# Attention's cluster chain on DVE in three pieces, x rows turned a head later; an expert up projection with the weights stationary and 256 tokens moving

## The reference, cut to what matters

```python
# attention: batch 2, 8 heads, 768 positions, 64 dims, 16 clusters per head
q_assign = argmax(einsum(q_n, c_n)); k_assign = argmax(einsum(k_n, c_n))
mask = q_assign[:, :, :, None] == k_assign[:, :, None, :]
scores = where(mask, scale * q @ k.T, -1e9)
x = softmax(scores) @ v                      # rearranged to (1536, 512)
# dense block: d_model 512, d_ff 1024
h = x @ w_in
solu = h * softmax(h)
x = (layernorm(solu) * g_ln) @ w_out
# experts: 8 experts, w1 (512, 1024), w2 (1024, 512), top 1, capacity 384
expert_idx = argmax(x @ w_gate); gate_w = softmax(x @ w_gate)[expert_idx]
h = maximum(disp @ w1, 0)
y = h @ w2
out[i] = gate_w[i] * y[expert_idx[i], pos[i]]
```

## Time and profile before

| | |
|---|---|
| median of 3 runs | 747.68 us (745.71 to 748.03) |
| the profiled execution, its own time | 743.6 us |
| its span | 741.8 us |
| mean granted TensorE clock | 0.956 |
| PE, DVE, ACT, POOL busy, share of the span | 86%, 60%, 56%, 39% |
| bytes by DMA, mean rate | 86.08 MB, 116 GB/s |
| the costliest DVE groups | p_lo 192 of 547 ns, maximum 96 of 954 ns |

### The profile page before, as it was taken

One profiled execution on the slowest core, in us unless ns is written; L12 is line 12 of the kernel. 1 busy time (PEld: TensorE's weight loads), 2 busy tenths in 40 slices (PEclk: granted clock), 3 DMA queues, 4 the chain that ended last, 5 costly groups with the idle time before them and its releaser, 6 DMA issues. The chain is left out here.

```text
span 741.8 us, 12378 instructions
## 1 busy us (share of the span) xinstructions
PE 640.7 (86%) x4272; PEld 560.7 (76%) x4272; DVE 444.5 (60%) x773; ACT 418.6 (56%) x772; POOL 292.4 (39%) x277
## 2 busy tenths in 40 slices
PE   2888999999999899579999999734999999999983
PEld 2778888888888889468888888633777887877862
DVE  5688887888788788346656465351635616346430
ACT  3577877787778788435453545310645627446630
POOL 3457676667767656464332010003022312314211
PEclk9999999999999999789999999975999999999997
DMA  4745454545454530071120000007547535367200
GB/s 119 206 118 151 120 152 116 132 117 151 108 142 102 136 87 2 15 271 42 43 85 14 28 15 15 28 15 258 172 164 274 191 129 208 125 237 248 73 18 14
DMA packets 37378, 86.08 MB, mean 116 GB/s; under 512 B 6719, under 2 KB 8895, under 8 KB 37314
## 3 DMA queue, kind: packets, MB, share of 16 engines
q1 hardware_dynamic: 33474, 75.78, 34.4%
q0 software_dynamic: 3840, 9.45, 3.9%
HBM read 53.74 MB, written 12.58 MB: 89 GB/s over the span
## 5 line engine op out<-in xcount | busy, mean ns | idle before, releaser
L437 DVE TENSOR_TENSOR p_lo<-t_ps,p_hi 128x384 f16<-128x384 f32 x192 | 103.7, 547 | 17.4 <-ACT p_hi L328 15.5
L432 DVE TENSOR_REDUCE neg_max<-s_ps 128x1 f32<-128x768 f32 x96 | 91.6, 954 | 32.4 <-PE s_ps L531 31.9
L328 ACT ACTIVATE p_hi<-t_ps 128x384 f16<-128x384 f32 x192 | 89.9, 488 | 31.9 <-PE t_ps L542 29.3
L531 PE MATMUL s_ps<-KK,QQ 128*128 128x384 f32 x384 | 94.0, 368 | 0.0
L554 PE MATMUL pv_ps<-v_cut,p_hi 128*128 128x192 bf16 x576 | 91.5, 248 | 0.7 <-ACT pv_sb L328 0.5
L542 PE MATMUL t_ps<-consts,p_exp 128*128 128x128 f32 x576 | 90.8, 277 | 1.4 <-ACT p_exp L352 0.8
L1238 POOL DMA_INDIRECT out<-y,info x24 | 26.5, 1105 | 164.3 <-ACTq L1179 78.3
L555 PE MATMUL pv_ps<-v_cut,p_lo 128*128 128x128 bf16 x576 | 89.1, 221 | 0.0
L352 ACT ACTIVATE p_exp<-s_ps,neg_max 128x768 f32<-128x768 f32 x96 | 87.0, 906 | 1.7 <-DVE neg_max L432 1.7
L542 PEld LDWEIGHTS t_ps<-consts,p_exp 128*128 128x128 f32 x576 | 71.7, 146 | 7.9 <-issue 2.4
L531 PEld LDWEIGHTS s_ps<-KK,QQ 128*128 128x128 f32 x384 | 65.2, 197 | 0.2 <-issue 0.2
(11 more groups left out here) (199 smaller groups left out, 1575.4 us busy)
## 6 DMA issues: line engine op xcount, KB each, us to landing
w_raw<-in_w SPq DMA_DIRECT2D x36, 512.0 KB, 4.9
x_t<-in_w SPq DMA_DIRECT2D x28, 512.0 KB, 8.0
QQ<-qk_hi SPq DMA_DIRECT2D x32, 192.0 KB, 3.2
KK<-qk_hi SPq DMA_DIRECT2D x32, 192.0 KB, 3.7
qk<-in_qT SPq DMA_DIRECT2D x16, 192.0 KB, 4.0
qk<-in_kT SPq DMA_DIRECT2D x16, 192.0 KB, 4.3
QQ<-qk_lo SPq DMA_DIRECT2D x16, 192.0 KB, 4.0
KK<-qk_lo SPq DMA_DIRECT2D x16, 192.0 KB, 4.0
```

What stands on the lines that cost most here:

```text
L328: return nc.scalar.activation(out, in_, ACT.Copy, **kw)
L432: V.tensor_reduce(neg_max[:, g % PB:g % PB + 1], both(s_ps[g % 2]), AX.XY, ALU.max, negate=True).then_inc(max_done, 1)
L437: V.tensor_tensor(p_lo[g % PB][:, TH * i:TH * (i + 1), :], t_ps[i][:, 0:HALF].rearrange("p (k q) -> p k q", q=P), p_hi[g % PB][:, TH * i:T ...
L531: ins = mm(s_ps[g % 2][:, i, 0:HALF], QQ[s][:, j, P * t:P * (t + 1)], KK[s][:, j, HALF * i:HALF * (i + 1)], start=j == 0, stop=j == 1)
```

## The change

In the attention `clusters` is cut into `tops` (first two instructions), `firsts` (next two) and `marks` (the two compares), which DVE runs behind tiles 2, 3 and 4 of the head. `turn_one_hot` and `mask_rows_out` move from tile 3 to tile 5. `pair_of` now puts the turning of pair n into tiles 3 and 4 of head 2n + 3; three waits are added or changed in PE's stream so that `misc` is not overwritten.

In the experts the two first tiles of an expert are one up projection: w1 is stationary, in 128 by 128 blocks, and 256 tokens move. Its result is h already turned, so `turn_h`, `relu` and `rectify` go. ACT writes ht_hi with the ReLU in the copy, bank by bank, and DVE writes ht_lo with a maximum in the subtraction. A third tile (`up_extra`) has 128 tokens moving. The pair is always computed, even where an expert holds one tile. PE's order is: x of the third slot turned if it holds tokens, up_pair(e), x of the next expert's two tiles turned, up_extra(e) if held, down of each held tile. An empty third slot is no longer turned. There are 4 `x_in` buffers and 7 raw buffers, in the space of `x_t`, and ACT and DVE cut the next expert's weights between the banks of the current one. The diff, cut to its core:

```diff
-            if h >= 2 and h % 2 == 0 and T - 2 <= t < T:
-                return h // 2 - 1, t - (T - 2)
+            if h >= 3 and h % 2 == 1 and TH <= t < TH + 2:
+                return (h - 3) // 2, t - TH
...
-                    if t == 3 and h + 2 < HEADS:
+                    if t == T - 1 and h + 2 < HEADS:
...
-                    if t == 2 and h + 2 < HEADS:
-                        clusters(h + 2)
+                    if h + 2 < HEADS:
+                        if t == 2:
+                            tops(h + 2)
+                        if t == 3:
+                            firsts(h + 2)
+                        if t == 4:
+                            marks(h + 2)
...
                     pe.wait_ge(mask_out, min(2 * n + 5, HEADS))
+                    if 2 * n + 5 < HEADS:
+                        pe.wait_ge(pick, PICK * (2 * n + 5) + 2)
+                    if n >= 1:
+                        pe.wait_ge(xt_out, 2 * n)
...
-                        if h >= 3 and h % 2 == 1:
-                            pe.wait_ge(xt_out, 2 * ((h - 1) // 2))
+                        if h >= 4 and h % 2 == 0:
+                            pe.wait_ge(xt_out, h - 2)
                         logits(h + 2, 0, TH)
                     if t == 1 and h + 2 < HEADS:
                         logits(h + 2, TH, T)
-                    if t == 3 and h + 2 < HEADS:
-                        turn_one_hot(h + 2)
                     if pair_of(h, t):
                         turn_x(*pair_of(h, t))
+                    if t == T - 1 and h + 2 < HEADS:
+                        if h >= 3 and h % 2 == 1:
+                            pe.wait_ge(xt_out, h - 1)
+                        turn_one_hot(h + 2)
...
+            def pair_high(e, b):
+                act.wait_ge(pair_full, BANKS * e + b + 1)
+                if e >= 1:
+                    act.wait_ge(y_full, CT * (e - 1) + 2)
+                copy(of_bank(ht[0], b, PAIR), bank(b, PAIR), ACT.Relu).then_inc(pair_hi, 1)
...
+            def extra_high(e, b):
+                act.wait_ge(extra_full, EXTRA * e + b + 1)
+                if e >= 1:
+                    act.wait_ge(y_full, CT * e)
+                copy(of_bank(ht_extra[0], b, P), bank(b, P), ACT.Relu).then_inc(extra_hi, 1)
...
+                g = CT * e
+                with holds(act, bits, g + 2):
+                    x_high(g + 2)
+                with act.Else():
+                    pass_over(act, xs_hi_done)
+                for b in range(BANKS):
+                    cut_hi(e + 1, b)
+                    pair_high(e, b)
+                if e + 1 < E:
+                    x_high(g + CT)
+                    x_high(g + CT + 1)
+                with holds(act, bits, g + 2):
+                    for b in range(EXTRA):
+                        extra_high(e, b)
+                with act.Else():
+                    pass_over(act, extra_hi, EXTRA)
+                cut_hi(e + 1, 4)
+                cut_hi(e + 1, 5)
+                weigh(g)
+                cut_hi(e + 1, 6)
+                cut_hi(e + 1, 7)
+                for t in range(1, CT):
+                    with holds(act, bits, g + t):
+                        weigh(g + t)
...
+            def rectified_rest(out, in_, high):
+                return V.scalar_tensor_tensor(out, in_, 0.0, high, ALU.max, ALU.subtract)
+
+            def pair_low(e, b):
+                dve.wait_ge(pair_hi, BANKS * e + b + 1)
+                rectified_rest(of_bank(ht[1], b, PAIR), bank(b, PAIR), of_bank(ht[0], b, PAIR)).then_inc(pair_lo, 1)
...
+            def up(e, b, x, width, signal):
+                w = w1[e % 2]
+                for i in range(512 // width):
+                    f = 512 // width * b + i
+                    n = 0
+                    for c in range(KC):
+                        for wp, xp in ((0, 0), (0, 1), (1, 0)):
+                            ins = mm(h_ps[b][:, width * i:width * (i + 1)], w[wp][:, c, P * f:P * (f + 1)],
+                                     x[xp][:, c, :], start=n == 0, stop=n == 3 * KC - 1)
+                            n += 1
+                ins.then_inc(signal, 1)
+
+            def up_pair(e):
+                pe.wait_ge(xs_lo_done, CT * e + 2)
+                if e >= 1:
+                    pe.wait_ge(w_lo, PW * (e - 1) + PIECES_OF_W)
+                    pe.wait_ge(extra_lo, EXTRA * e)
+                for b in range(BANKS):
+                    if e >= 1:
+                        pe.wait_ge(pair_lo, BANKS * (e - 1) + b + 1)
+                    up(e, b, xs, PAIR, pair_full)
+
+            def up_extra(e):
+                pe.wait_ge(xs_lo_done, CT * e + 3)
+                for b in range(EXTRA):
+                    pe.wait_ge(pair_lo, BANKS * e + b + 1)
+                    up(e, b, xs_extra, P, extra_full)
...
+                    if t == 0 and c % 2 == 0:
+                        pe.wait_ge(pair_lo, BANKS * e + c // 2 + 1)
+                    if t == 2 and c == 0:
+                        pe.wait_ge(extra_lo, EXTRA * (e + 1))
+                    for hp, wp in ((0, 0), (0, 1), (1, 0)):
+                        h = ht_extra[hp][:, c, :] if t == 2 else ht[hp][:, c, P * t:P * (t + 1)]
+                        ins = mm(y_ps[g % 2][:, :], h, w[wp][:, c, :], start=n == 0, stop=n == 3 * FC - 1)
...
             for e in range(E):
-                for t in range(CT):
-                    g = CT * e + t
-                    if t == 0:
-                        up(g)
-                        turn_next(g + 2)
-                        if e > 0:
-                            last_stage(pe, bits, e - 1, CT - 1, y_full, down)
-                        turn_h(g)
-                    else:
-                        with holds(pe, bits, g):
-                            up(g)
-                            turn_next(g + 2)
-                            down(g - 1)
-                            turn_h(g)
-                        with pe.Else():
-                            turn_next(g + 2)
-                            pass_over(pe, h_full, ht_full)
-            last_stage(pe, bits, E - 1, CT - 1, y_full, down)
+                g = CT * e
+                with holds(pe, bits, g + 2):
+                    turn_x(g + 2)
+                with pe.Else():
+                    pass_over(pe, xt_full)
+                up_pair(e)
+                if e + 1 < E:
+                    turn_x(g + CT)
+                    turn_x(g + CT + 1)
+                with holds(pe, bits, g + 2):
+                    up_extra(e)
+                with pe.Else():
+                    pass_over(pe, extra_full, EXTRA)
+                down(g)
+                for t in range(1, CT):
+                    with holds(pe, bits, g + t):
+                        down(g + t)
+                    with pe.Else():
+                        pass_over(pe, y_full)
...
-            more_raw = [flat[:, win[0].shape[2] * r:win[0].shape[2] * (r + 1)] for r in range(4)]
-            experts(nc, a, info, mask, x2_dram, ((w1_first, w2_first), (win, wout)), raw + more_raw, consts, const_at, tiles_per_expert)
+            FF = win[0].shape[2]
+            more_raw = [flat[:, FF * r:FF * (r + 1)] for r in range(3)]
+            rows = [flat[:, 3 * FF + DM * r:3 * FF + DM * (r + 1)] for r in range(6)]
```

More of the change, by code:

```diff
@@ L406, in _, with tops @@
             V = nc.vector
-            def clusters(h):
+            def tops(h):
                 k = PICK * h
@@ L428, in clusters @@
                                     best[:, :, s].unsqueeze(2).to_broadcast([P, T, C]), op).then_inc(pick, 1)
+            def clusters(h):
+                tops(h)
+                firsts(h)
+                marks(h)
             def maximum(g):
@@ L1110, in _, with experts @@
             dve.drain()
-def experts(nc, a, info, mask, x2_dram, weights, raw, consts, const_at, tiles_per_expert):
+def experts(nc, a, info, mask, x2_dram, weights, raw, x_in, y, consts, const_at, tiles_per_expert):
     E, DM, FF = a["w1"].shape
@@ L1131, in experts @@
     RAW = len(raw)
+    PAIR = 2 * P
+    BANKS = FC * PAIR // 512
+    EXTRA = FC * P // 512
     with ExitStack() as ctx:
@@ L1175, in holds, with pass_over, piece, x_part @@
             return eng.If((bits & (1 << g)) > 0)
-        def pass_over(eng, *done):
-            for signal in done:
+        def pass_over(eng, signal, times=1):
+            for _ in range(times):
                 eng.drain().then_inc(signal, 1)
[L1181 to L1191, removed]
-            if t == 0:
[L1194 to L1200, removed]
+        def piece(e, j):
+            return PW * (e - 1) + j
+        def x_part(p, g):
+            t = g % CT
+            return xs_extra[p][:, :, :] if t == 2 else xs[p][:, :, P * t:P * (t + 1)]
+        def turned(g):
+            return xt_ps[g % 2][:, :].rearrange("p (c t) -> p c t", c=KC)
+        def of_bank(x, b, width):
+            n = 512 // width
+            return x[:, n * b:n * (b + 1), :]
+        def bank(b, width):
```

(35 more changed lines are left out.)

148 lines of the change are left out of this document (49 added, 99 removed).

## The result

After the change the kernel takes 725.14 us (median of four runs, 723.98 to 726.12); the kernel before, run beside it, 746.69. The ratio is 0.9713 [0.9686, 0.9741], faster. The forecast was 729.0 in a range of 717 to 742. The profiled execution took 726.12 us with a span of 724.3, against 743.6 and 741.8 before: 17.5 us less span, where the prediction had 18.7. (By the medians the kernel is 21.6 us shorter; the profiled execution before was near the fast end of its executions.)

What follows compares the result with a forecast made beforehand. It took TensorE, DVE and ACT as almost level in the attention and TensorE alone as the bound in the experts. Terms -10.5, -4.1, -5.1 and +1.0 sum to -18.7, from 747.7 to 729.0 us, range 717 to 742.

Steps and rivals of the forecast that it cites:

- Cluster chain: Attention: split in three pieces, with later one-hot transposes, it saves 0.75 us a head in 14 heads, 10.5 us.
- x rows: Attention: turning x in tiles 3 and 4 of odd heads is covered by TensorE's wait for DVE; six pairs gain 4.1 us.
- Clock: Attention: with shorter idle stretches three drops of TensorE's granted clock go, 1.7 us each, 5.1 us; bounds 0 and 5.1.
- Experts: Expert stage: narrower matmuls cost about what no longer turning h saves; all terms sum to 1.0 us slower.
- (a): Rival, experts' up projection: the weight load alone sets the pair's pace, 0.112 us a matmul; 721.3 us; chance 0.12.
- (c): Rival, experts' up projection: 256 columns run no faster than 384, 0.178 us a matmul; 772 us; chance 0.07.
- Skipped parts: Experts: 13 times a skipped part drains TensorE, 0.9 us each, 11.7 against 13.6 before, a gain of 1.9.
- The first up: Experts: the first up projection waits for the second tile's rest until 517.6 and not 516.2, costing 1.4 us.
- The gather's stall: Experts: the gather of expert 2's third tile lands some 2 us after TensorE wants it, costing 2 us once.
- (b): Rival, attention: the chain's pieces cost more than counted, no gain from the split, clock still falls; 744.6 us; chance 0.10.
- my bound from below: Attention, cluster chain: the pieces could cost their full 2.83 us, making each head 0.9 us slower.
- (d): Rival, experts: skipping the third tile's 96 matmuls costs a code fetch, seven at 3.1 us, 22 us; 751 us; chance 0.04.

Runs made afterwards that it cites:

- e3: Changed kernel, but POOL waits for the head's reciprocal before it cuts the dense weights; 719.85 us, ratio 0.9651 to the kernel before.
- e4: Changed kernel with DVE's whole cluster chain in one piece behind tile 2, one-hot transposes still behind tile 5; 758.07 us, ratio 1.0151.
- e6: Changed kernel with DVE's addition of 1e-9 to the denominators replaced by a tensor_reduce that only copies them; 719.0 us, ratio 0.96.
- e7: Changed kernel with POOL's wait for the reciprocal, and without the multiplication by rank in the cluster chain; 716.44 us, ratio 0.9596.
- e2: Experts of the changed kernel with the attention of the kernel before; 745.41 us, ratio 0.9989.
- e1: Attention of the changed kernel with the experts of the kernel before; 727.79 us, ratio 0.975.
- e5: Changed kernel with POOL's wait for the reciprocal, and an expert's third tile gathered one step of POOL's loop earlier; 717.11 us, ratio 0.9593.

## Why the prediction held, step by step

**Cluster chain: too little was expected of it, and its side effect was missed.** Heads 1 to 15 without the collision gained 258.0 - 234.0 = 24.0 us. Of that, 5.0 are the clock's (below) and 4.1 x, if it is taken at its predicted size; 14.9 are left for the chain in 13 heads, 1.15 each and not 0.75. Periods are 16.0, not 16.4. DVE's timeline in e3 says where the difference lies: from maximum to maximum the three tiles take 2.46, 2.60 and 2.37 us instead of the 2.58, 3.09 and 2.59 that I had added up from the earlier trace rows. And TensorE's waits for a p_lo in e3 are 0.2 at most from 75 to 265 us, where the prediction had 0.3 and 0.8.

```profile
148.79 0.95 DVE L444 TENSOR_REDUCE neg_max<-s_ps 128x1 f32<-128x768 f32 x1
...
150.12 0.50 DVE L421 TENSOR_TENSOR lg_eq<-lg_eq,consts 128x192 f32<-128x192 f32 x1
150.66 0.35 DVE L424 TENSOR_REDUCE lg_rank<-lg_eq 128x12 f32<-128x192 f32 x1
...
151.39 0.95 DVE L444 TENSOR_REDUCE neg_max<-s_ps 128x1 f32<-128x768 f32 x1
...
152.72 0.54 DVE L434 TENSOR_TENSOR one_hot<-lg_eq,lg_rank 128x96 bf16<-128x96 f32 x2
```

That is 0.83 less of DVE's time a head, of which 0.4 showed in the period. The rank multiplication takes 0.50 and not 0.85, the two comparisons 0.54 and not 0.86, together 0.67 of it. These durations were no property of the instructions. In e4, with the chain back in one piece, they are 0.84 and 0.86 again (DVE's timeline of e4):

```profile
172.07 0.84 DVE L420 TENSOR_TENSOR lg_eq<-lg_eq,consts 128x192 f32<-128x192 f32 x1
...
173.33 0.86 DVE L433 TENSOR_TENSOR one_hot<-lg_eq,lg_rank 128x96 bf16<-128x96 f32 x2
```

For the multiplication the rows show a wait for POOL; these are the instructions of POOL that it met, in before and in e3:

```profile
160.00 1.00 POOL L277 TENSOR_TENSOR pv_sb<-pv_sb 128x384 f32<-128x384 f32 x1
```

```profile
149.91 0.50 POOL L259 CAST v_cut<-v_raw 128x384 bf16<-128x384 f32 x1
```

Before: POOL ends at 161.00, the multiplication at 160.36 + 0.85 = 161.21. In e3: 150.41 and 150.62. Both times it ends 0.21 us after POOL. The Trainium skill ("SBUF — State Buffer", Who interferes with whom) has the rule: a VectorE instruction with two SBUF inputs contends with a GpSimd one that reads SBUF. These rows agree with it. No run moves POOL's instruction away from the multiplication alone, so here the cause rests on these ends and not on an experiment as in e3 and e6. **The step that failed** is thus that durations were carried from one place to another as constants and that POOL was named only as a queue: at the new places the chain's pieces got shorter (14.9 - 13 x 0.75 = 5.1 us of period in all), and the addition on the denominators, which the change doesn't touch, got 2.3 us longer in six heads and made after's heads 6.3 longer in all. The two errors nearly cancel, and so do two others: head 0 took 2.0 longer and the experts, with 0.2 before their first up, ended 1.6 shorter instead of 1.0 longer. That the total came out well is in part this luck.

**x rows.** Confirmed as far as it shows: in e3 heads with and without x are equally long, in e7 they are not. Half of the 0.69 for a pair shows in before: head 1, in front of which no x is turned, lasts 17.18 and the other odd heads about 17.5. The 4.1 us were not measured alone.

**Clock.** Three drops were to go, 5.1 us. Heads 5, 9 and 12 of before were 1.6, 1.6 and 1.8 us longer than their neighbours, 5.0 together, and after has none: granted clock 1.00 from 75 to 265.

**Head 0** had no term of its own, only the 0.75 of the 14 heads. After's takes 2.0 us more than before's, but that is scatter from run to run and not the change: with the attention of before it took 15.21 in one profiled run and 17.27 in another (e2), with that of after 17.18 and 14.86 (e1). The scores' matmuls show it, before and after:

```profile
28.44 0.95 PE L531 MATMUL s_ps<-KK,QQ 128*128 128x384 f32 x4
```

```profile
28.64 1.63 PE L547 MATMUL s_ps<-KK,QQ 128*128 128x384 f32 x4
```

In the profiled executions with a longer head 0 they take nearly twice as long for some microseconds. The clock's column of the windows reads 1.00 there, so what slows them stays open. In e3, e5 and e7 all of them run at the short duration, as in the profiled run of before, and head 0 takes 13.2 to 13.3 against 15.21: where nothing slows the matmuls, the new order makes head 0 about 1.9 shorter, and in the profiled run of after this was hidden.

**Experts: the zero was right, the terms less so.** A pair of tiles lasts 11.75 us in the chain above, 0.1224 a matmul, predicted 0.122; 96 matmuls of the single third tile go from 568.07 to 578.84, 10.77, predicted 10.8. (Two roundings in the prediction change nothing: the router's pace is 2.63 / 12 = 0.22 and not 0.21, and 1.78 + 0.2 - 1.2 is 0.78 and not 0.75.) Rivals (a) and (c), a pace of 0.112 or 0.178, are out. Three small terms were off. Skipped parts cost 4.8 + 2.6 = 7.4 us, not 11.7; they were priced by waits of the earlier trace rows that held more than the jump. The first up began 0.2 later and not 1.4, and spent 1.3 at the lower clock where before had 1.8. The gather's stall was 2.7 as a wait, and its pair, from 554.17 to the end at 567.23, took 1.3 more than 11.75 for the clock that the wait cost: 4.0 and not 2.0. These corrections sum to -4.3 - 1.2 - 0.5 + 2.0 = -4.0, which with the +1.0 forecast would be -3.0; measured were 0.2 before the first up, -1.8 from there on, and a ratio of 0.9989. 1.4 us are not explained, and are less than what the stretch scatters by: the same experts take 211.6 in e2 and 213.8 in e4.

**The rivals.** (b), pieces that cost more than counted, did not come. e4 shows what it would have been like: the full 2.83 us in one piece make even heads 0.5 longer than in before, within the 0.9 of my bound from below, but odd heads 2.0 longer, because the clock falls in every one of them, and for that the bound had nothing. The expectation of e4 left out the same term, and with a delay of 2.06 for the 2.47 measured it fell 21 us short. A chain in one piece sits in front of a p_lo that TensorE wants at once, so the slack of later tiles can't help it. (d), a code fetch behind each skip, is out: 0.46 us behind a skip of 96 matmuls (539.48), and none of the 13 over 0.9.

## What to carry to other kernels

A duration read from a timeline belongs to its place: on DVE and POOL it can hold the other engine's time, so compare the shortest and the longest of the same instruction before you carry its mean to another place, and look at what the other engine runs there. A chain on an in-order queue costs the bottleneck engine what exceeds the slack *in front of the next thing it waits for*; pieces smaller than that slack are nearly free, one long piece is not, wherever its consumer is moved. When a stage gets shorter, look for instructions that newly meet: here six such meetings took back a quarter of the gain, and one wait, or another form of the instruction, returned it.

## What the runs showed of the hardware

- A DVE addition of 0.16 us took up to 2.52 when it met POOL's subtraction of 2.36, and ended with it; as a reduction it took 0.15 in the same place. The reciprocal beside it was never slowed (0.19).
- The addition was held by a POOL instruction whose recorded start came 0.01 to 0.13 us after its own. All six times POOL's instruction before that one was still running when the addition began. Where a scaling of the dense weights or a cast came next on POOL in after, the addition was done 0.03 to 0.20 us after the running one (146.27 behind 146.24, 179.53 behind 179.34). Why it gets in there and not before the subtraction stays open.
- From 75 to 265 us, a wait of TensorE of 2.0 us in the odd heads of e4 is followed by some four microseconds at a granted clock of about 0.65, and the longer waits of 2.3 in its even heads are not; nor are the waits of 0.9 in after. The length of the wait alone doesn't decide.
- Matmuls of 256 columns of this type run at 0.122 us, of 128 columns at 0.112, with a new weight load for each: a moving operand of 128 columns costs nearly as much as one of 256.
